# Attention and two feed-forward layers on one core: stage 1 as one straight program, and its DVE, ACT and POOL work dealt out again

## What is computed

```python
# attention: softmax(scale * q k^T + bias, masked to 8 global and 96 local keys) @ v
# first layer, x is (1536, 512), w_in (512, 1024), w_out (1024, 512)
h = x @ w_in
solu = h * softmax(h)
ln = (solu - mean(solu)) / sqrt(var(solu) + 1e-6) * g_ln
y = ln @ w_out
# second layer, w_gate and w_val (512, 1536), w_out (1536, 512)
yn = y / sqrt(mean(y * y) + 1e-6) * rms_g
out = (silu(yn @ w_gate) * (yn @ w_val)) @ w_out
```

## Time and profile before

| | before |
|---|---|
| median of 3 runs | 586.67 us (586.62 to 586.96) |
| the profiled execution | 585.97 us, its span 584.2 us |
| PE busy, matmuls | 539.8 us, 92% of the span |
| PE busy, weight loads | 462.2 us, 79% |
| DVE busy | 453.6 us, 78% |
| ACT busy | 283.5 us, 49% |
| POOL busy | 143.8 us, 25% |
| mean granted TensorE clock | 0.977 |

### The profile page before, as it was taken

How to read it: one execution, slowest core, us unless ns; L and a number is a source line. 1 busy time by engine, 2 the same in 40 slices (tenths; PEclk the granted TensorE clock), 3 DMA queues, 4 the chain that set the end, 5 groups by cost and what they waited for, 6 DMA issues and landing times.

```text
span 584.2 us, 10632 instructions
## 1 busy us (share of the span) xinstructions
PE 539.8 (92%) x3481; PEld 462.2 (79%) x3481; DVE 453.6 (78%) x949; ACT 283.5 (49%) x625; POOL 143.8 (25%) x259
## 2 busy tenths in 40 slices
PE   1796999999998999995979799999999999999997
PEld 1565777777776777774879799999999999999996
DVE  4769878877986878885797977787697787787765
ACT  3668566776677687743755422332242242242221
POOL 4541222123233343334624503003003003000000
PEclk9996899999999999996999899999999999999999
DMA  8656343443354253021412021001102102100013
GB/s 216 196 149 182 109 122 83 127 126 109 89 169 137 77 160 106 4 89 54 143 38 73 1 70 40 1 8 66 37 1 72 36 0 72 36 0 1 6 68 144
DMA packets 24833, 46.99 MB, mean 80 GB/s; under 512 B 2908, under 2 KB 9064, under 8 KB 24792
## 3 DMA queue, kind: packets, MB, share of 16 engines
q1 hardware_dynamic: 24480, 46.48, 26.9%
q10 hardware_dynamic: 312, 0.01, 0.0%
HBM read 40.18 MB, written 6.29 MB: 80 GB/s over the span
## 4 chain that ended last, share of the span: by engine, by line
PE 72%; DVE 17%; issue 4%; POOL 3%; ACT 2%; DMA 1%; DVEq 0%; ACTq 0%; SPq 0%; POOLq 0%
PE hidden L459 9%; PE hidden L460 9%; PE hidden L461 9%; PE turned L459 3%; PE turned L461 3%; PE turned L460 3%; PE mixed L1554 3%; PE scores_a L460 3%; PE scores_a L459 3%; PE scores_b L459 3%; PE scores_b L461 3%; PE scores_b L460 3%; PE scores_a L461 3%; PE turned L1539 2%; PE scores_a L1526 2%
## 5 line engine op out<-in xcount | busy, mean ns | idle before, releaser
L890 ACT ACTIVATE acts<-gate 128x512 fp32r<-128x512 f32 x36 | 22.8, 634 | 130.0 <-DVE gate L1343 120.6
L794 ACT ACTIVATE probs_t<-turned 116x512 f32<-116x512 f32 x48 | 28.7, 597 | 58.5 <-PE turned L1539 58.5
L459 PE MATMUL hidden<-down_hi,acts 128*128 128x512 f32 x144 | 56.5, 393 | 0.0
L460 PE MATMUL hidden<-down_lo,acts 128*128 128x512 f32 x144 | 56.5, 392 | 0.0
L461 PE MATMUL hidden<-down_hi,acts 128*128 128x512 f32 x144 | 56.3, 391 | 0.0
L1358 DVE TENSOR_TENSOR out_acc<-hidden,out_acc 128x512 f32<-128x512 f32 x60 | 41.4, 690 | 11.8 <-PE hidden L461 10.3
L784 ACT ACTIVATE probs<-logits,neg_max 128x232 f32<-128x232 f32 x96 | 45.6, 480 | 6.0 <-DVE neg_max L1185 6.0
L459 PE MATMUL hidden<-in_hi,xt_hi 128*128 128x512 f32 x96 | 44.3, 461 | 1.1 <-DVE xt_lo L1208 0.9
L459 PE MATMUL turned<-yt_hi,w_hi 128*128 128x256 f32 x144 | 41.3, 287 | 3.5 <-DVE yt_lo L1290 3.5
L733 POOL TENSOR_TENSOR sums<-w_raw 128x512 f32<-128x512 f32 x5 | 6.9, 1383 | 142.9 <-DMA w_raw<-w_val 142.9
L461 PE MATMUL turned<-yt_hi,w_lo 128*128 128x256 f32 x144 | 41.1, 286 | 0.0
(11 more groups left out here) (185 smaller groups left out, 1663.3 us busy)
## 6 DMA issues: line engine op xcount, KB each, us to landing
qk_raw<-qk_pairs SPq DMA_DIRECT2D x96, 180.0 KB, 3.2
v_in<-v_windows SPq DMA_DIRECT2D x12, 448.0 KB
y_spill<-y_out SPq DMA_DIRECT2D x12, 256.0 KB, 4.2
y_in<-y_spill SPq DMA_DIRECT2D x6, 512.0 KB, 4.7
w_raw<-w_gate SPq DMA_DIRECT2D x6, 512.0 KB, 3.7
w_raw<-w_val SPq DMA_DIRECT2D x6, 512.0 KB, 4.7
down_raw<-w_down SPq DMA_DIRECT2D x6, 512.0 KB, 3.7
out<-out_acc SPq DMA_DIRECT2D x12, 256.0 KB, 2.0
```

The costliest lines, as they stand in the source:

```text
L459: pe.matmul(acc, hi, other_hi, start=first, stop=False)
L460: pe.matmul(acc, hi, other_lo, start=False, stop=False)
L794: nc.scalar.activation(probs_t[:, p % 2], turned[0:HALF, :], ACT.Copy).then_inc(probs_t_ready, 1)
L890: nc.scalar.activation(act_hi[:, half].rearrange("p f n -> p (f n)"), gate[:, half], ACT.Copy).then_inc(act_rounded, 1)
```

## The change

The loop of stage 1 is gone: t = -1 to 11 are written out on every engine, and the counting of semaphores by registers with it. `bias_even` and its copies are gone, `take_logits` reads `bias` directly. Then the work is dealt out in another way.

- `apply_norm` moves from DVE (one operation of 128x1024) to ACT (two of 128x512, `ACT.Identity` with a scale and a bias from `col`). PE may turn the first half when that half is done. POOL makes the bias, one operation more in `newton`.
- `normalise_y` moves from DVE to ACT (two operations of 128x512 for each pair of tiles).
- `sum_y` moves from POOL to DVE for all three blocks. `sum_w(0)` moves from POOL to DVE and is spread over (5, 1), (5, 2), (5, 3) and (6, 0), t and p; the weights are loaded at t = 4 into a buffer of their own, `w0_raw`. The sums of the other five groups of weights stay on POOL.
- `turn_y` and `scale_y` of the tiles 0 to 3 stand in t = 5 to 8, one in each. Those of the tiles 4 to 7 all stand in t = 11. `scale_y` stands ahead of `copy_turned` on ACT, and `copy_y` too.
- The RMS factor is made for five groups of tiles (`groups_of_y`) in columns of their own.
- SP issues `load_y(3)` in part 1 of t = 11, and `load_w(1)` behind `load_y(5)`.

```diff
-        turn_at = {(7, 0): 0, (7, 1): 1, (8, 0): 2, (8, 1): 3, (11, 3): 4}
-        round_y_at = {(8, 2): 0, (8, 3): 1, (9, 0): 2, (9, 1): 3, (9, 2): 4, (9, 3): 5, (10, 0): 6}
...
-        NORMALISE_AT = {(6, 3): 0, (7, 3): 1, (10, 3): 2, (11, 2): 3}
-        SCALE_AT = {(6, 0): 0, (6, 3): 1, (7, 3): 2, (10, 3): 3, (11, 3): 4}
+        turn_at = {(5, 0): 0, (6, 0): 1, (7, 0): 2, (8, 0): 3, (11, 0): 5, (11, 1): 6, (11, 3): 7}
+        scale_y_at = {(5, 1): 0, (6, 1): 1, (7, 1): 2, (8, 1): 3, (11, 0): 5, (11, 1): 6, (11, 3): 7}
+        normalise_at = {(5, 0): 0, (7, 0): 1, (10, 3): 2, (11, 1): 3}
+        round_y_at = {(8, 0): (0, 1), (9, 0): (2, 3), (9, 1): (4,), (10, 0): (5, 6)}
+        split_y_at = {(8, 1): 0, (8, 2): 1, (9, 2): 2, (9, 3): 3, (10, 0): 4, (10, 1): 5, (10, 2): 6}
+        sum_y_at = {(8, 3): P7, (9, 0): P5, (9, 1): P6, (9, 2): P4}
+        sum_w_at = {(5, 1): P7, (5, 2): P5, (5, 3): P6, (6, 0): P3}
+        round_w_at = {(11, 0): (0, 1, 2), (11, 1): (3, 4), (11, 2): (5, 6)}
...
+        newton_y_after = {3: (0,), 5: (1,), 9: (2,), 10: (3,), 11: (4,)}
+        groups_of_y = ((0, 2), (2, 4), (4, 8), (8, 10), (10, 12))
...
             def load_w(j):
-                if is_first(j):
-                    sp.wait_ge(yt_split, PRODUCTS)
-                else:
+                if known(j) and j == 1:
+                    sp.wait_ge(yt_split, 2 * PRODUCTS)
+                elif not is_first(j):
                     sp.wait_ge(w2_split, PRODUCTS * j)
...
+                pool.tensor_scalar(col[:, 7:8], col[:, 4:5], col[:, 1:2], None, ALU.mult
+                                   ).then_inc(newton_steps, 1)
                 pool.wait_ge(newton_steps, NEWTON_STEPS * (t + 1))
+                pool.tensor_scalar(col[:, 8:9], col[:, 7:8], moments[:, 0:1], -1.0, ALU.mult, ALU.mult
                                    ).then_inc(rstd_ready, 1)
...
+            def apply_norm(t):
+                act.wait_ge(rstd_ready, t + 1)
+                for n in range(N1):
+                    here = slice(n * BANK, (n + 1) * BANK)
+                    nc.scalar.activation(gated[:, here], gated[:, here], ACT.Identity, bias=col[:, 8:9],
+                                         scale=col[:, 7:8]).then_inc(ln_ready, 1)
...
+            def sum_y(b, i):
...
+                if i == P7:
+                    dve.wait_ge(yt_scaled, 4 * (b + 1))
+                    nc.vector.tensor_tensor(added[P7], y22, y12, ALU.subtract).then_inc(yt_summed, 1)
...
             def turn_ln(t, n):
+                pe.wait_ge(ln_ready, N1 * t + n + 1)
                 if n == 0:
...
-                    turned_y = {6: 2, 7: 4, tiles - 1: 8}
-                    if known(t) and t in turned_y:
+                    turned_y = {4: 1, 5: 2, 6: 3, 7: 4, 10: 7, 11: 8}
+                    if t in turned_y:
                         pe.wait_ge(yt_scaled, turned_y[t])
...
-            for t in range(-AHEAD, LOOP_FROM):
+            for t in range(-AHEAD, tiles):
                 one_tile(t, t % 2)
-            with pe.Fori(LOOP_FROM // 2, LOOP_TO // 2) as i:
-                for even in range(2):
-                    one_tile(2 * i + even, even)
-            for t in range(LOOP_TO, tiles):
-                one_tile(t, t % 2)
```

More of the change, by code:

```diff
@@ L842, in scale_y, with normalise_y @@
                 ins.then_inc(yt_scaled, 1)
+            def normalise_y(u):
+                act.wait_ge(y_newton_steps, Y_NEWTON_STEPS * (group_of[u] + 1))
+                act.wait_ge(y_loaded, 16 * (u + 1))
+                for i in range(2):
+                    ins = nc.scalar.activation(y_in[u][:, i], y_in[u][:, i], ACT.Copy,
+                                               scale=rstd[:, 1, 2 * u + i:2 * u + i + 1])
+                ins.then_inc(yn_ready, 1)
+            def apply_norm(t):
[4 more added lines that the diff above has]
+                                         scale=col[:, 7:8]).then_inc(ln_ready, 1)
             def round_y(b, place):
@@ L915, in one_tile @@
                         exp_hidden(t)
+                    if p == 1 and is_tile(t - DRAIN):
+                        copy_y(t - DRAIN, even)
+                    if p < 2 and (t, p) in scale_y_at and t < tiles - 1:
+                        scale_y(scale_y_at[t, p])
+                    if p < 3 and (t, p) in normalise_at:
+                        normalise_y(normalise_at[t, p])
+                    for place in round_y_at.get((t, p), ()):
+                        round_y(0, place)
                     copy_turned(n, p)
@@ L979, in _ @@
             nc.scalar.activation(silu_warm[:], sum_sq[:, 0:1], ACT.Silu)
-            scale_y(5)
-            scale_y(6)
+            normalise_y(4)
             copy_1(0)
-            scale_y(7)
             copy_y(tiles - 2, 0)
+            round_y(1, 0)
+            round_y(1, 1)
             take_silu(0, 0)
-            round_y(1, 0)
+            apply_norm(tiles - 1)
+            round_y(1, 2)
             round_ln(tiles - 1, 0)
-            round_y(1, 1)
+            round_y(1, 3)
             round_ln(tiles - 1, 1)
-            for place in range(2, PRODUCTS):
+            for place in range(4, PRODUCTS):
                 round_y(1, place)
@@ L1449, in _ @@
                 general_attention()
-            for t in range(-AHEAD, LOOP_FROM):
+            for t in range(-AHEAD, tiles):
                 one_tile(t, t % 2)
-            with dve.Fori(LOOP_FROM // 2, LOOP_TO // 2) as i:
-                for even in range(2):
-                    one_tile(2 * i + even, even)
-            for t in range(LOOP_TO, tiles):
-                one_tile(t, t % 2)
+            for i in (P7, P5, P6, P4):
+                sum_y(1, i)
             gate_1(0)
-            apply_norm(tiles - 1)
             sum_u2(0)
-            normalise_y(4)
             split_y(1, 0)
@@ L1489, in _ @@
             add_out(0, 0, 1)
-            split_y(2, 2)
+            for i in (P7, P5):
+                sum_y(2, i)
             val_1(1)
             gate_value(1, 0)
+            for i in (P6, P4):
+                sum_y(2, i)
             gate_2(1)
             split_act(1, 0)
-            for place in range(3, 5):
+            for place in range(2, 5):
                 split_y(2, place)
@@ L1687, in one_tile @@
                         continue
-                    first = known(t) and t == 0
+                    first = t == 0
                     score_pair(n + 1, (p + 1) % pairs)
@@ L1706, in one_tile @@
                         turn_ln(t - 1, 1)
+                    if t == tiles - 1 and p == 0:
+                        turn_y(4)
                     if p == 0 and is_tile(t - 2):
```

340 lines of the change are left out of this document (151 added, 189 removed).

## The result

The changed kernel is slower: 590.79 us, median of 4 runs (590.29 to 591.35), against 586.66 for the kernel before beside it. The ratio is 1.007, with a 95% interval of 1.0054 to 1.0086. The forecast was 581.4. The profiled execution has a span of 588.5 where the kernel before had 584.2.

The account below looks back on a forecast made before the run. PE was taken to set the time, so gains could come only where it waits or runs at the lower clock. The terms summed to -5.3 from 585.97 profiled: 580.7, or 581.4 as a median, range 576.5 to 585.6.

Parts of the forecast that it names:

- LN by ACT, every tile: Normalisation on ACT: no wait at the first transposition, 0.15 at the second in 9 tiles, +1.4; +0.7 in t = 1.
- sign of being wrong: Plain tiles of over 20 us in place of 19.7, with waits for ACT at turned_x<-gated, would show a mis-sized term.
- Rivals A: All is gained: the clock doesn't fall again, LN by ACT and DVE sums are hidden; 576.7, chance 0.22.
- Rival C: Slower: LN by ACT misses PE's first transposition in each of 10 tiles; 588.0 at 0.8 a tile, chance 0.08.
- The loop: Stage 1 written out: register counting is hidden behind PE, at most 0.4 to gain; with the bias copies -0.2.
- t = 7 and 8: PE's waits there for ACT and for qk_hi of DVE all go: -3.5, bounds 1.8 and 3.9.
- t = 11, first wait: Newton steps begin earlier, but ACT's row lets PE turn LN only 2.0 earlier: -2.9, with new waits of +0.9.
- t = 11, second wait: PE's wait near 296 for ln_lo of tile 11 falls from 3.05 to 0.8: -2.2.
- The clock: Of 3.0 us lost to the lower clock in t = 11, 1.7 is lost again: -1.3, bounds 0 and -3.0.
- DVE sums: Token and weight sums on DVE: seven operations ahead of recip_wide and qk_hi cost 0.2 each, +1.5, bounds 0 and 4.8.
- Last block: Token block 2: PE waits 0.7 for normalise_y(5), the 3.47 wait for yt_lo stays in substance; +0.3, bounds -1.5 and +2.5.
- Rival B: POOL's sums of weights 1 slow DVE's token sums, mostly at the wait at 329: +2.1 to +4.2, chance 0.12.

Follow-up runs that it names:

- exp_first: The changed kernel with apply_norm still on ACT, but behind exp_pair in part 1 and not ahead of it: 583.04 us, ratio 0.9942 to the kernel before.
- before_straight: The kernel before with its loop over t = 2 to 5 written out on every engine, and nothing else: 584.96 us, ratio 0.9973.
- norm_dve: The changed kernel with apply_norm back on DVE as one 128x1024 operation, without POOL's operation for the bias: 576.87 us, ratio 0.9835 to the kernel before.
- w_sums_late: norm_dve with the four sums of the first weights back on POOL, behind the Newton steps of tile 9: 577.16 us, ratio 0.9836 to the kernel before.

## Why the prediction was wrong

**The step that failed is "LN by ACT, every tile":** +1.4, with +0.7 for t = 1, where 13.9 was measured. The mechanism, an operation on ACT that makes PE's transpositions late, was named in it; its sizes were too small, and one way of losing was not seen. The prediction's own sign of being wrong, plain tiles of over 20 us, is there: 20.2.

- *"The first half is done at about 143.65, ahead of PE's 143.93: no wait."* The two operations took 1.52 and PE was served 0.87 after the first began; the group mean is 0.81 (below), where I took 0.63 and 0.71. With the factor 0.37 later and only 0.21 of room, PE starts 0.25 later there each time (0.92 a tile less the 0.67 below).

```profile
L814 ACT ACTIVATE gated<-gated,col 128x512 f32<-128x512 f32 x24 | 18.2, 806 | 15.2 <-POOL col L658 15.2
```

- *"That is a new wait of up to 0.3 a tile; where no other late step is in it I expect half."* It is 0.67 at the second transposition of each plain tile, 2.95 behind the first in place of 2.28. The sum did have `exp_pair` behind the normalisation, but `round_ln` began 1.50 behind PE's transposition where it had 1.27 (145.2 against 143.93), and it let PE start at the end of `ln_lo`, where 0.15 lie between them (109.88 and 110.03 above); with its 0.3 that makes 0.68. Rivals A and C called ACT's idle time of 1.85 room. Most of it, 1.17 in the changed kernel, is the wait for POOL that the normalisation needs, and in this order `exp_pair` waits through it as well; exp_first shows that the order is more than half of the loss. Halving was wrong too: PE, busy for 59.62 of 60 us, had nowhere to make such a wait good, and the 0.67 stands in full in each tile.
- Some tiles pay more: 2.2 in t = 1 (forecast 0.7), where a piece of `w_out` is rounded between `exp_pair` and `round_ln`, and 1.5 in t = 8 and 9, where POOL's chain is longer by a further 0.34 beside DVE's token sums. The sum had one price for all but t = 1.
- The upper bound (10 x 0.6 = 6) was built on the same operation times, and so the range missed too. Rival C had the sign but not the place: it was about the first transposition alone, with a decision from 0.67 a tile. That wait is 0.25; the second makes 0.67; together 0.92.

**The loop, -0.2, was -2.0.** *"In 100 to 160 ... PE idles for 0.4 us in all"* was taken as the most that could be gained. But the tiles t = 2 to 4 are 1.3 shorter in before_straight, more than the 0.4 of idle time in the whole window, which is 0.0 there. A delay of a quarter microsecond hardly shows as idle time of PE; distances from start to start show it. With this the plain tile's reference was 19.28, not the 19.7 from which I read PE's wish times, and the net change of 0.5 a tile in the trace hid a loss of 0.9. What in DVE's loop is slow is not tried.

**The rest of the sum was near, partly by luck.** Against before_straight, norm_dve is all the other parts of the change: 8.1 us faster, where my terms make 7.2.
- t = 7 and 8: forecast -3.5. Over t = 4 to 8, with four transpositions in other places and the weight sums in, it is -4.5 in the table.
- t = 11, first wait: the forecast had PE there 2.0 earlier, and the column t = 10 of norm_dve is 2.0 shorter. But ACT's row was added up with `apply_norm` in it, 1.25, which norm_dve hasn't; in its place ACT stands idle for 0.75 while PE turns a y tile, which the sum left out. In the changed kernel, for which the sum was made, the column is only 0.9 shorter. ACT's row took 9.5 there (forecast 9.4) and PE's two waits 1.62 and 1.87 (forecast 1.9 and 1.8), but the row began 12.1 behind `turn_ln(9, 0)` in place of the 11.3 of the forecast, 0.6 of it for the later second transposition of tile 9.

```profile
273.12 0.65 PE L1617 MATMUL turned_x<-ident,y_in 128*128 128x128 f32 x4 [1.62 <-ACT y_in L806]
275.64 0.63 PE L1588 MATMUL turned_x<-ident,gated 128*128 128x128 f32 x4 [1.87 <-ACT staging L798]
```

- t = 11, second wait: forecast -2.2; from `turn_ln(10, 0)` to the second transposition of tile 11 it is 18.68 + 4.81 = 23.49 in before_straight and 19.00 + 2.07 = 21.07 in norm_dve, -2.4.
- The clock: forecast -1.3 with a short dip in t = 11. In the changed kernel the two waits of t = 11 left it at 1.00 (the first window below, of the changed kernel, in which PE is busy for 2.83 of 6.64). A dip came later, around the wait of tile 11 (the second window): 0.26 x 6.5 = 1.7 lost in place of 3.0. The size was right, the place not. norm_dve, with waits of 1.61 and 1.32 in t = 11, does have its dip there (the third window, of norm_dve). And the reading of the kernel before left one out: the clock is at 0.50 behind the wait of 3.47 at 329 as well (the last window, of the kernel before), and it was not behind the one of 3.05. So the length of a wait alone doesn't tell here what the clock does.

```profile
271.36:278.00 6.64, 2.83 (x15) 1.86 (x14) 2.12 (x5) 5.67 (x13) 0.30 (x1) 1.00 0.36 120
293.50:300.00 6.50, 5.42 (x33) 5.41 (x34) 2.70 (x5) 4.58 (x8) 0.18 (x1) 0.74 0.00 0
```

```profile
263.76:267.17 3.41, 3.41 (x10) 2.73 (x11) 2.58 (x4) 1.47 (x3) 0.00 (x0) 0.50 0.25 93
```

```profile
329.02:332.00 2.98, 2.98 (x14) 2.98 (x15) 2.98 (x4) 0.57 (x2) 1.08 (x1) 0.50 0.00 0
```

- DVE sums: forecast +1.5; 0.6 in t = 9 and 0.5 in t = 5 (norm_dve against w_sums_late), and no less on POOL.
- Last block: forecast +0.3, and this was far too small. From the second transposition of tile 11 to the end it is 289.7 in before_straight and 290.3 in norm_dve, but before_straight has two dips of the clock there (0.54 over 292.7 to 296.4, 0.50 over 327.1 to 330.5) and norm_dve one (0.57 over 318.0 to 322.0). The kernel before, with the one at 329 alone, takes 288.0: 2.2 less than norm_dve.

Rival B was at work inside that last term. I gave it a price on top of an unchanged wait; the wait (3.17 in the changed kernel, 3.26 in norm_dve) looked unchanged, but 1.5 of it were this meeting. The Trainium skill, page "SBUF — State Buffer", section "SBUF: two separate sides", says that a DVE operation with two SBUF inputs and a GpSimd operation that reads SBUF exclude each other, and that the one that starts later waits for the whole of the other. This case's traces agree, with 1.67 for 0.69 on DVE beside POOL operations of 1.3 to 1.6. The copy with one input (1.33 for 0.43) was held up as well. For one input the page has such a wait only in certain modes of DVE, and no run here shows in which mode the copy ran.
